# Attention in a fused attention, experts and SwiGLU kernel: a tile's scores in three 384-column blocks instead of two of 512 and a remainder

## The reference, cut to what matters

```python
q_pool = q.reshape(B, H, S // 2, 2, D).mean(axis=3)      # 4 x 8 heads, 576 rows, D = 64
scores = np.matmul(q_pool, k.transpose(0, 1, 3, 2)) / np.sqrt(D)    # 576 x 1152 per head
attn = np.exp(scores - scores.max(-1, keepdims=True))
attn = attn / (attn.sum(-1, keepdims=True) + 1e-09)
x = np.matmul(attn, v)                                   # 576 x 64 per head
```

## Time and profile before

| | |
|---|---|
| device time, three runs | 1533.62, 1538.85, 1537.81 us, median 1537.81 |
| span of the profiled execution, first to last instruction | 1528.9 us |
| PE busy in the span | 1423.7 us (93%) |
| DVE, ACT, POOL busy | 56%, 45%, 33% |
| a pair of heads in the steady stage | 38.94 us |
| engines' busy time in such a pair (38.90 us) | PE 38.05, DVE 30.90, ACT 31.44, POOL 18.73 |
| mean granted TensorE clock in the span | 0.977 of full |

### The profile page before, as it was taken

How to read it: one execution, slowest core, us unless ns; L and a number is a source line. 1 busy time by engine, 2 the same in 40 slices (tenths; PEclk the granted TensorE clock), 3 DMA queues, 4 the chain that set the end, 5 groups by cost and what they waited for, 6 DMA issues and landing times.

```text
span 1528.9 us, 25832 instructions
## 1 busy us (share of the span) xinstructions
PE 1423.7 (93%) x8085; PEld 1234.6 (81%) x8086; DVE 856.1 (56%) x1603; ACT 685.2 (45%) x1635; POOL 500.0 (33%) x336
## 2 busy tenths in 40 slices
PE   4999999999999999974897999996999999999998
PEld 3788888888888888753786788885999999999997
DVE  4787787777777778856343344453643232323222
ACT  4888888888888887751214301101521111111111
POOL 2844444444444422057729702202201010110000
PEclk8999999999999999996998999998999999999999
DMA  7221111111111121145527612113521010000000
GB/s 254 89 69 50 48 51 54 54 54 54 54 54 54 54 65 56 50 152 201 192 96 231 222 41 96 55 41 106 157 68 35 7 35 7 34 7 21 0 21 21
DMA packets 86122, 115.16 MB, mean 75 GB/s; under 512 B 8768, under 2 KB 47680, under 8 KB 86080
## 3 DMA queue, kind: packets, MB, share of 16 engines
q1 hardware_dynamic: 70160, 72.66, 15.1%
q10 hardware_dynamic: 12880, 31.99, 6.2%
q0 software_dynamic: 3040, 9.96, 1.9%
HBM read 87.33 MB, written 27.26 MB: 75 GB/s over the span
## 4 chain that ended last, share of the span: by engine, by line
PE 44%; POOL 5%; issue 5%; DVE 2%; DMA 1%; ACT 0%; SPq 0%; DVEq 0%; POOLq 0%
POOL w_parts L1024 4%; PE ps_g L1729 3%; PE ps_g L1731 3%; PE ps_g L1730 3%; PE ps_out L1746 3%; PE ps_out L1745 3%; PE ps_v L1731 3%; PE ps_v L1730 3%; PE ps_v L1729 3%; PE ps_out L1744 3%; PE ps_y L1427 2%; PE ps_y L1429 2%; PE ps_y L1428 2%; PE ps_h L1402 2%; PE ps_h L1404 2%
## 5 line engine op out<-in xcount | busy, mean ns | idle before, releaser
L639 DVE TENSOR_TENSOR p_lo<-ps_t,p_hi 128x512 fp32r<-128x512 f32 (+1 forms) x336 | 221.2, 670 | 82.0 <-ACT p_hi L500 78.7
L500 ACT ACTIVATE p_hi<-ps_t 128x512 fp32r<-128x512 f32 (+1 forms) x336 | 193.3, 585 | 73.0 <-PE ps_t L688 71.1
L564 DVE TENSOR_REDUCE maxima<-ps_s 128x1 f32<-128x512 f32 x288 | 196.4, 683 | 34.2 <-PE ps_s L795 32.1
L1024 POOL TENSOR_TENSOR w_parts<-raw_w,w_parts 128x1024 fp32r<-128x1024 f32 x64 | 150.9, 2394 | 186.9 <-ACT w_parts L1079 186.7
L524 ACT ACTIVATE probs<-ps_s,neg_max 128x512 f32<-128x512 f32 x288 | 200.1, 695 | 15.6 <-DVE neg_max L577 15.5
L688 PE MATMUL ps_t<-ident,probs 128*128 128x128 f32 x1296 | 191.5, 273 | 0.0
L688 PEld LDWEIGHTS ps_t<-ident,probs 128*128 128x128 f32 x1296 | 156.6, 140 | 33.3
L1620 ACT ACTIVATE silu<-ps_g 128x384 f32<-128x384 f32 x72 | 35.4, 491 | 315.2 <-PE ps_g L1731 315.2
L795 PE MATMUL ps_s<-kq_t 128*128 128x512 f32 x512 | 169.6, 413 | 4.2 <-ACT probs L524 2.3
L1079 ACT ACTIVATE w_parts<-raw_w 128x1024 fp32r<-128x1024 f32 x64 | 66.9, 1058 | 218.4 <-PE ps_h L1404 104.9
L1673 DVE TENSOR_TENSOR silu<-ps_g,silu 128x384 f32<-128x384 f32 x72 | 40.1, 557 | 210.9 <-ACT silu L1620 210.9
(11 more groups left out here) (194 smaller groups left out, 3233.5 us busy)
## 6 DMA issues: line engine op xcount, KB each, us to landing
raw_w<-in_moe_w ACTq DMA_DIRECT2D x61, 512.0 KB, 3.7
raw_k<-in_k SPq DMA_DIRECT2D x16, 576.0 KB, 4.0
raw_v<-in_v SPq DMA_DIRECT2D x16, 576.0 KB, 3.8
raw_q<-in_q SPq DMA_DIRECT2D x32, 256.0 KB, 4.0
x_by_slot<-zeros SPq DMA_DIRECT2D x1, 6400.0 KB, 20.1
y_by_slot<-x_out SPq DMA_DIRECT2D x25, 256.0 KB, 2.0
x_all<-x_by_slot SPq DMA_DIRECT2D x23, 256.0 KB, 2.7
out<-o_row SPq DMA_DIRECT2D x18, 256.0 KB, 2.2
```

What stands on the lines that cost most here:

```text
L500: nc.scalar.activation(p_hi[m % PT][:, 0:w], T[ring(kind, j)][:, 0:w], ACT.Copy).then_inc(hi_ready, 1)
L564: nc.vector.reduce_max(maxima[:, 3 * tile + h:3 * tile + h + 1], S[(2 * tile + h) % SR][:, :], AX).then_inc(max_done, 1)
L639: nc.vector.tensor_tensor(p_lo[m % PT][:, 0:w], t[:, 0:w], p_hi[m % PT][:, 0:w].bitcast(F32), ALU.subtract).then_inc(t_free_dve, 1)
L1024: nc.gpsimd.tensor_tensor(w_part(n, parity, 1, at, PIECE), raw[j % RAW][:, :], w_part(n, parity, 0, at, PIECE).bitcast(F32), ALU.subtract) ...
```

## The change

Scores of a tile are made in three blocks of 384 columns (`BLK`), each in a PSUM bank of its own, three banks side by side out of four. Even tiles of a pair (odd ones in every second pair) use banks 0 to 2, the others 1 to 3. The bank that the tile before does not use, 0 or 3, takes the next tile's first block (`scores_early`); the other two blocks (`scores_late`) go to banks 1 and 2, which the tile before uses too, and wait until its exponential is done. One activation takes the exponential of all 1152 columns and one row sum. DVE reduces the early block by itself, and the two late ones in one instruction.

```diff
-    SCORES_AT, MAXIMA_AT, EXP_AT = (0, 1), (0, 1), (0, 0, 1)
+    SCORES_AT, MAXIMA_AT, EXP_AT = (0, 1), (0, 1), 0
-        S = [ps(f"ps_s{i}", 512) for i in range(SR)]
-        R = ps("ps_r", 512)
+        S = ps("ps_s", 4 * 512)
+        def s_bank(par, tile):
+            return (par + tile) % 2
+        def s_blocks(first, count):
+            return S[:, first * 512:(first + count) * 512].rearrange("p (b c) -> p b c", c=512)[:, :, 0:BLK]
# ACT: one exponential where there were exp_half 0, exp_rem and exp_half 1
+                    to = probs[:, tile * SK:(tile + 1) * SK].rearrange("p (b c) -> p b c", c=BLK)
+                    nc.scalar.activation(to, s_blocks(s_bank(par, tile), 3), ACT.Exp,
                                          bias=neg_max[:, tile:tile + 1],
+                                         accum_out=sums[par][:, sum_col(tile)]).then_inc(exp_done, 1)
# DVE: maxima
+                def largest_early(p, par, tile):
+                    dve.wait_ge(s_ready, 2 * TILES * p + 2 * tile + 1)
+                    bank = 0 if s_bank(par, tile) == 0 else 3
+                    nc.vector.reduce_max(maxima[:, 2 * tile:2 * tile + 1], S[:, bank * 512:bank * 512 + BLK], AX
+                                         ).then_inc(max_done, 1)
+                def largest_late(p, par, tile):
+                    dve.wait_ge(s_ready, 2 * TILES * p + 2 * tile + 2)
+                    nc.vector.tensor_reduce(maxima[:, 2 * tile + 1:2 * tile + 2], s_blocks(1, 2), AXY, ALU.max
+                                            ).then_inc(max_done, 1)
+                    dve.wait_ge(max_done, 2 * TILES * p + 2 * tile + 2)
+                    nc.vector.tensor_reduce(neg_max[:, tile:tile + 1], maxima[:, 2 * tile:2 * tile + 2], AX, ALU.max,
                                             negate=True).then_inc(bias_ready, 1)
# DVE, once a pair: the sum over three partial row sums goes
-                    s3 = sums[1 - par][:, :].rearrange("p (t s) -> p t s", s=3)
-                    nc.vector.reduce_sum(total[:, :], s3, AX).then_inc(norm_chain, 1)
-                    nc.vector.tensor_scalar(total[:, :], total[:, :], 1e-9, None, ALU.add
+                    nc.vector.tensor_scalar(total[:, :], sums[1 - par][:, :], 1e-9, None, ALU.add
# PE: scores and scores_rem go
+                def scores_early(p, par, tile, opening):
+                    if not (opening and tile <= 1):
+                        pe.wait_ge(exp_done, TILES * p + tile - 1)
+                    if tile == TC:
+                        pe.wait_ge(c_padded, p + 1)
+                    block(par, tile, 0 if s_bank(par, tile) == 0 else 2).then_inc(s_ready, 1)
+                def scores_late(p, par, tile, opening):
+                    if not (opening and tile == 0):
+                        pe.wait_ge(exp_done, TILES * p + tile)
+                    for i in (1, 2) if s_bank(par, tile) == 0 else (0, 1):
+                        last = block(par, tile, i)
                     last.then_inc(s_ready, 1)
-                                scores(*nxt, 1)
-                                if nxt[2] % QT == 0:
-                                    scores_rem(*nxt)
+                                scores_late(*nxt, kind == "first" and tile < TC)
```

More of the change, by code:

```diff
@@ L11 @@
 AX = mybir.AxisListType.X
+AXY = mybir.AxisListType.XY
 P = 128
@@ L196, in attention @@
         stack2 = sb("stack2", [P, D])
-        maxima = sb("maxima", [P, 3 * TILES])
+        maxima = sb("maxima", [P, 2 * TILES])
         neg_max = sb("neg_max", [P, TILES])
-        sums = [sb(f"sums{i}", [P, 3 * TILES]) for i in range(2)]
+        sums = [sb(f"sums{i}", [P, TILES]) for i in range(2)]
         total = sb("total", [P, TILES])
@@ L501, in take, with exps @@
                                          ).then_inc(hi_ready, 1)
[L503 to L507, removed]
-                                         bias=neg_max[:, tile:tile + 1],
[L509 to L526, removed]
+                def exps(p, par, kind, tile):
+                    act.wait_ge(bias_ready, TILES * p + tile + 1)
+                    if kind != "first" and tile == 0:
+                        act.wait_ge(t_filled, before(p, kind, every))
+                    if kind != "first" and tile == QT:
+                        act.wait_ge(t_filled, upto(p, kind, every, UNIT_LAST["b"]))
+                    if kind != "first" and tile == TC:
+                        act.wait_ge(t_filled, upto(p, kind, every, UNIT_LAST["c"]))
+                    to = probs[:, tile * SK:(tile + 1) * SK].rearrange("p (b c) -> p b c", c=BLK)
+                    nc.scalar.activation(to, s_blocks(s_bank(par, tile), 3), ACT.Exp,
+                                         bias=neg_max[:, tile:tile + 1],
+                                         accum_out=sums[par][:, sum_col(tile)]).then_inc(exp_done, 1)
                 def body(p, par, kind):
@@ L535, in body @@
                                 j += 1
[L536 to L541, removed]
+                            if kind != "tail" and n == EXP_AT:
+                                exps(p, par, kind, tile)
                 def first_parts(p):
@@ L799, in scores_rem, with block @@
-                def scores_rem(p, par, tile, waits=True):
-                    if waits:
-                        pe.wait_ge(exp_rem_done, TILES * p + tile)
-                    for t in range(QT if tile < TC else 1):
-                        ops = operands(par, tile + t)
-                        for n, (w, head) in enumerate(ops):
-                            at = (head * CH + CH - 1) * P
-                            last = nc.tensor.matmul(R[:, t * P:(t + 1) * P], w, kq_t[par][:, at:at + P],
-                                                    start=(n == 0), stop=(n == len(ops) - 1))
-                    last.then_inc(r_ready, 1)
+                def block(par, tile, i):
+                    ops = operands(par, tile)
+                    bank = s_bank(par, tile) + i
+                    for n, (w, head) in enumerate(ops):
+                        at = head * CH * P + i * BLK
+                        last = nc.tensor.matmul(S[:, bank * 512:bank * 512 + BLK], w, kq_t[par][:, at:at + BLK],
+                                                start=(n == 0), stop=(n == len(ops) - 1))
+                    return last
```

64 lines of the change are left out of this document (18 added, 46 removed).

## The result

| | before | after |
|---|---|---|
| device time, median (range) | 1535.71 us (1531.28 to 1538.85, 4 runs) | 1584.44 us (1581.48 to 1586.50, 4 runs) |
| ratio, 95% interval | | 1.0313 [1.0295, 1.0331] |
| span of the profiled execution | 1528.9 us | 1579.7 us |
| a steady pair of heads, mean of six | 38.89 us | 41.74 us |

What follows compares the result with a forecast made beforehand. PE sets the attention's pace, chained tile by tile with ACT and DVE; late blocks would wait for the whole exponential. Full pairs +42.6, last +3, first +5, together +50: span 1528.9 to 1579, plus 8.9 gives 1588 us, range 1545 to 1620.

Steps and rivals of the forecast that it cites:

- The late blocks behind a wait: PE's late score matmuls in a slot: 0.80 us when PE has waited, 0.70 without, since weights are not loaded ahead.
- the line for the exponential: ACT, per tile: fixed part plus 0.84 ns a column gives 1.23 us for 1152 columns, bounds 1.16 and 1.77.
- the line for the maximum: DVE, late blocks: 1.05 ns a column gives 0.95 us for 768 columns in one reduction, bounds 0.85 and 1.10.
- PE works less: PE in attention: 384-column blocks without remainders save 1.0 us a pair, 16 us in all, if nothing waits.
- The path 0.71 + 0.50 + 1.36: Slot's first fill to ACT's copy, to the exponential, to PE getting the banks: 2.57 us against PE's own work of 2.17 at most.
- Slot by slot: New lengths of a pair's nine slots: changes from -0.38 (slot 8) to +0.78 us (slot 1), together +3.04.
- The sum: Attention: 14 full pairs +42.6 us, last pair about +3, first pair +5; together +50 us.
- The first pair: Opening pair, hardly any steps to cover the 3.5 us loop from late blocks to exponential: +3 to +7, taken as +5 us.
- the 8.9 us: Whole kernel: median of the runs stands 8.9 us above the profiled span, added to 1579 for 1588 us.
- The covered case: Rival: exponential ends before PE arrives, so only PE's saving is left, -16 us, 1522; chance 0.09.
- a partial cancelling: Rival: waits half as long because unburdened ACT starts exponentials 0.2 to 0.3 us earlier; +5 to +20, around 1550; chance 0.12.
- The clock: Rival: PE's short idles put a tenth of the attention at 1.2 GHz, +60 us more, 1648; chance 0.06.

Runs made afterwards that it cites:

- the last versions: Changed kernel with three 384-column exponentials, shared banks first, own bank's behind the second step: 1538.72 us; with the late maximum also in two reductions: 1535.76 us.

## Why the prediction was right

**The sizes.** The late blocks behind a wait (0.81 us against 0.80), the line for the exponential (1.23 against 1.221) and the line for the maximum (0.95 against 0.952) all came out. The Trainium skill's figure ("VectorE: DVE Perf Modes", the section on the TRN2 errata) gives 1.10 us for such an exponential; the measured 1.221 decides, and one instruction over three banks has no extra price here. That PE works less did not show in the time.

**The path 0.71 + 0.50 + 1.36.** It measures 0.72 + 0.49 + 1.36, so that the late blocks start 2.57 us into slot 1. The weakest step, the distance from fill to exponential, held.

**Slot by slot.** The slots begin as the prediction counts them. In the order 5, 6, 7, 8, 0, 1, 2, 3, 4 the slots last 5.79, 3.49, 4.68, 3.48, 4.83, 4.28, 6.10, 5.78 and 3.31 us (the first from 339.68, 0.43 behind the fill at 339.25; merged rows count 0.36 for their first fill). The forecast had 5.87, 3.48, 4.65, 3.57, 4.87, 4.28, 6.22, 5.81 and 3.23. None is off by more than 0.12; the sum is 41.74 against 41.98.

**The sum.** 14 pairs by the measured 41.74 - 38.89 = 2.85 us make 39.9 (forecast 42.6). The first pair's last late blocks come at 63.94 us against 58.49: +5.5 (forecast +5, from pieces at the full clock). The routing's first transposes start at 707.97 against 659.34, +48.6 in all, so the last pair and the tail took 3.2 (forecast 3). The remaining 2.2 us of the span's +50.8 lie behind the attention, in stages that the change does not touch; I have no cause for them, and single executions of the changed kernel differ by up to 5 us. The forecast of 1588 was built on the median of the runs, 1537.81, plus 50, so the wrong reading of the 8.9 us did no harm: by medians the step was 48.7 us.

The first pair's number is in part luck. Its clock differs from before, which the forecast had left alone. Stretches of 4 us, first before, then after (PE's busy time comes first, the granted clock behind POOL's):

```profile
38.00:42.00 4.00, 3.38 (x21) 2.69 (x21) 2.39 (x5) 3.76 (x13) 0.00 (x0) 1.00 1.05 360
42.00:46.00 4.00, 3.52 (x23) 2.60 (x22) 3.19 (x7) 3.19 (x11) 1.50 (x2) 1.00 0.24 57
```

```profile
38.00:42.00 4.00, 2.59 (x10) 2.28 (x10) 1.44 (x4) 1.52 (x3) 0.00 (x0) 0.50 1.03 358
42.00:46.00 4.00, 3.60 (x21) 3.03 (x20) 1.94 (x4) 2.81 (x5) 1.77 (x2) 0.74 0.21 48
```

Here the changed kernel has a second stretch at the lower level (0.50, 1.2 GHz), behind one in which PE was busy 1.99 of 4 us (34 to 38; that one was at 0.91, before the change at 0.57). From 22 us to the pair's end, 1 less the granted clock adds up to 6.8 us after and 5.1 before. So up to some 1.7 of the 5.5 us, an estimate, are clock and not waits.

**The rivals.** The covered case did not come, and a partial cancelling did not either: ACT has less to do, but it can't start before the fill. The clock stayed at 1.00 in the steady pairs of the changed kernel, with idle pieces of up to 1.0 us, and fell only in the opening pair. What the Trainium skill describes in "TensorE: Matmul & The Clock Gate", "A second HAM failure mode: psum-queue depth-cycling", a clock that goes up and down by short idles, these pairs do not show. In the kernel with the exponential one step later it was 0.93 in a stretch with waits near 2 us.

**The cause, as the runs show it.** Freeing the two shared banks earlier, with more instructions, gave back 23 us of 48; splitting the maximum by itself 7. The order on ACT, for which the forecast had no price, counts as much once the exponential is split: the second step's copy starts 0.7 us behind its fill when nothing holds it, 1.00 with two and 1.25 with three activations in front of it, and one instruction moved behind that copy gave 17 and 30 us. In the changed kernel slot 1's copy is not held (0.73), and moving or leaving out the own bank's exponential leaves PE's waits for `p_lo` at 18.2 and 17.5 us, where the changed kernel has 17.3; that is why the missing price did not spoil the number. Early release and right order together undo all but 3 to 6 us of the loss.

**What stays open.** The 16 us that PE should save by 384-column blocks without remainders never came out. In the last versions PE's weight loads still wait for `p_lo` (24.0 and 26.6 us in 540, against 9.1 before the change). With three exponentials and the move, slot 1's first product starts 0.71 us behind its fill, before the change 0.42, so at least a part is given back there; how much in all was not added up, and which part of the loop ACT copy, DVE rest, product sets that wait was not tried.

## What to carry to other kernels

Before merging instructions on an engine with slack, ask who waits for the first part of the old sequence and what stands behind it in the queue: the merged instruction gives up its buffers only at its end, and an item behind it that is ready waits for all of it. The price can be worked out ahead from one slot of the timeline, as start, release and the queue's own work up to there. Try a moved instruction by itself, since splitting gave 23 us with more work, and ordering another 17 with the same. Compare versions by a piece that repeats, as a pair does here within 0.1 us, where executions of one kernel differ by 5.

## What was not expected of the hardware

With the exponential one step late, PE's granted clock came to 0.93 and 0.97 in two stretches of 50 us (mean of the span 0.947), with PE busy 36.7 and 36.9 of 50 us and single waits of 1.96 us; in stretches of 4 us it went down to 0.57 and back to 1.00. In the steady pairs of the changed kernel, with waits up to 1.0 us and PE busy 93%, it was 1.00. So the long waits of that version came with a lower clock in the steady stage too, and the short ones of the changed kernel did not.
